# Another offset within 512 bytes for each split weight block of the second MoE

## The reference

```python
x = attention(q, k, v)          # 8 heads of 64, causal window of 128, ALiBi
x = soft_moe(x, phi, w1, w2)    # 32 slots: small products, all weights read once
# second MoE: every expert runs on every row
P = sinkhorn(exp(x @ w_gate - max), 8 rounds)
for e in range(8):
    h = np.maximum(x @ w1[e], 0.0)      # 512 -> 1024
    out += P[:, e:e + 1] * (h @ w2[e])  # 1024 -> 512
```

## Time and profile before

| what | value |
|---|---|
| median of 3 runs | 1057.57 us (1056.58 to 1058.82) |
| the profiled execution | 1057.44 us, its span 1055.5 us |
| mean granted TensorE clock | 0.969 of 2.4 GHz |
| TensorE matmul busy | 95% of the span |
| second MoE | from about 245 us to the end |

### The profile page before, as it was taken

The page is one execution under the profiler, slowest core; times in us unless marked ns, Lnnn a source line. Parts: engine busy times, 40 slices in busy tenths (PEclk is TensorE's granted clock), DMA queues, the critical chain, the costliest instruction groups (busy, mean ns, idle before and its releaser), DMA issues.

```text
span 1055.5 us, 25401 instructions
## 1 busy us (share of the span) xinstructions
PE 1005.1 (95%) x8599; PEld 924.3 (88%) x8599; DVE 748.2 (71%) x1994; ACT 583.7 (55%) x1368; POOL 615.1 (58%) x522
## 2 busy tenths in 40 slices
PE   7999979579999999999999999999999999999998
PEld 5888843029999999999999999999999999999998
DVE  7767741426898867876867778778768777877675
ACT  6777710224466746555655566466546564656552
POOL 6445410004487648684966596568747873877443
PEclk9999988658999999999999999999999999999999
DMA  5773267950200220022002200210040012000111
GB/s 184 262 277 112 71 273 265 408 209 2 81 1 2 81 81 2 2 82 81 2 3 83 81 2 2 99 63 1 14 148 5 2 72 91 2 2 20 61 41 61
DMA packets 36904, 87.81 MB, mean 83 GB/s; under 512 B 2976, under 2 KB 2976, under 8 KB 36768
## 3 DMA queue, kind: packets, MB, share of 16 engines
q1 hardware_dynamic: 36768, 86.07, 22.4%
HBM read 81.35 MB, written 4.72 MB: 82 GB/s over the span
## 4 chain that ended last, share of the span: by engine, by line
PE 41%; POOL 27%; issue 22%; DMA 4%; DVE 4%; ACT 1%; POOLq 1%; ACTq 0%; DVEq 0%
POOL s_split L499 19%; PE bank L775 8%; PE bank L777 7%; PE bank L779 7%; POOL t_split L504 4%; PE bank L568 3%; PE bank L578 3%; PE bank L597 3%; DMA late_raw<-slot_w_in 3%; PE bank L725 2%; PE bank L678 2%; PE bank L615 1%; POOL raw L533 1%; POOL raw L535 1%; POOL raw L537 1%
## 5 line engine op out<-in xcount | busy, mean ns | idle before, releaser
L499 POOL TENSOR_TENSOR s_split<-s_sum,s_split 128x512 fp32r<-128x512 f32 x288 | 372.5, 1309 | 342.2 <-ACT s_split L887 337.0
L1241 DVE SCALAR_TENSOR_TENSOR acc<-bank,gate_now,acc 128x256 f32<-128x256 f32 x441 | 228.6, 519 | 146.8 <-PE bank L779 145.8
L887 ACT ACTIVATE s_split<-s_sum 128x512 fp32r<-128x512 f32 x288 | 181.8, 632 | 247.6 <-PE bank L779 137.8
L775 PE MATMUL bank<-t_split,s_split 128*128 128x256 f32 x1008 | 284.2, 282 | 1.3 <-DVE acc L1235 1.1
L777 PE MATMUL bank<-t_split,s_split 128*128 128x256 f32 x1008 | 282.6, 280 | 0.0
L779 PE MATMUL bank<-t_split,s_split 128*128 128x256 f32 x1008 | 282.6, 280 | 0.0
L775 PEld LDWEIGHTS bank<-t_split,s_split 128*128 128x128 f32 x1008 | 189.4, 188 | 5.1 <-issue 3.4
L779 PEld LDWEIGHTS bank<-t_split,s_split 128*128 128x128 f32 x1008 | 192.6, 191 | 0.0
L777 PEld LDWEIGHTS bank<-t_split,s_split 128*128 128x128 f32 x1008 | 189.4, 188 | 0.0
L775 PE MATMUL bank<-t_split,a 128*128 128x256 f32 x576 | 164.1, 285 | 5.8 <-DVE acc L1235 2.5
L777 PE MATMUL bank<-t_split,a 128*128 128x256 f32 x576 | 162.6, 282 | 0.0
(11 more groups left out here) (167 smaller groups left out, 1952.5 us busy)
## 6 DMA issues: line engine op xcount, KB each, us to landing
raw<-big_w_in SPq DMA_DIRECT2D x15, 2048.0 KB, 8.6
early_raw<-slot_w_in SPq DMA_DIRECT2D x12, 1024.0 KB, 10.5
late_raw<-slot_w_in SPq DMA_DIRECT2D x10, 1024.0 KB, 13.5
slot_raw<-slot_w_in SPq DMA_DIRECT2D x7, 1024.0 KB, 5.2
q_ring<-q_tiles SPq DMA_DIRECT2D x18, 256.0 KB, 4.6
k_ring<-k_tiles SPq DMA_DIRECT2D x18, 256.0 KB, 4.9
v_ring<-v_rows SPq DMA_DIRECT2D x18, 256.0 KB, 2.7
out_rows<-acc SPq DMA_DIRECT2D x18, 256.0 KB, 2.0
```

Source lines behind the costliest of these rows:

```text
L499: pool.tensor_tensor(s_split[:, i, 1, :, :], s_sum[:, i, :, :], s_split[:, i, 0, :, :].bitcast(F32), ALU.subtract)\
L775: pe.matmul(to, left[:, 0, f, :], t_place(parity, k, 0)[:, f, :], start=(f == 0 and k in FRESH), stop=False, skip_group_check=k not in FRESH)
L887: act.activation(s_split[:, i, 0, :, :], s_sum[:, i, :, :], ACT.Copy).then_inc(s_hi_ready, 1)
L1241: done = dve.scalar_tensor_tensor(out=to, in0=got, scalar=gate, in1=to, op0=ALU.mult, op1=ALU.add)
```

## The change

Every block becomes a tensor of its own. In `t_split` each lies 16 floats (64 bytes) further than a gapless layout would have it, from `RAW_AT` itself on, so that the seven begin at 0, 64, 128, 192, 256, 320 and 384 bytes of the period. The three of `t_other` begin at 32, 288 and 480. No instruction, wait or shape changes: the same views are read and written at other addresses.

```diff
-        t_other, = place(OTHER_AT, RAW_AT, ("t_other", [P, len(DOUBLE), 2, HF, HD2], F32R))
-        t_split, = place(RAW_AT + PHASE, END + PHASE, ("t_split", [P, PRODUCTS, 2, HF, HD2], F32R))
+        BLOCK = 2 * HF * HD2
+        t_other = [place(OTHER_AT - PHASE + i * BLOCK + off, RAW_AT, (f"t_other{i}", [P, 2, HF, HD2], F32R))[0]
+                   for i, off in enumerate((8, 72, 120))]
+        t_split = [place(RAW_AT + i * (BLOCK + 16), END + PHASE, (f"t_split{i}", [P, 2, HF, HD2], F32R))[0] for i in range(PRODUCTS)]
...
             if i in DOUBLE and parity:
-                return t_other[:, DOUBLE.index(i), lo, :, :]
-            return t_split[:, i, lo, :, :]
+                return t_other[DOUBLE.index(i)][:, lo, :, :]
+            return t_split[i][:, lo, :, :]
```

## The result

| | kernel before | changed kernel |
|---|---|---|
| median | 1057.90 us (6 runs, 1056.02 to 1058.82) | 1063.67 us (6 runs, 1061.32 to 1067.61) |
| profiled execution | 1057.44 us, span 1055.5 | 1061.32 us, span 1059.3 |

The ratio is 1.0059, 95% interval 1.0039 to 1.0080: the changed kernel is slower, by 5.8 us at the median. Its runs spread over 6.3 us where those of before spread over 2.8, and the profiled execution is the lowest of them, so its trace shows 3.9 us of the 5.8.

What follows compares the result with a forecast made beforehand. TensorE's matmuls, one behind the other, were taken to bound the second MoE. Lost close stretches (2.4 us) plus wider spacing (4.5) made 6.9 us on 1057.44, giving 1064.3 us, range 1055 to 1082.

Steps and rivals of the forecast that it cites:

- both terms: The two nonzero parts of the sum: 2.4 us for lost close stretches and 4.5 us for wider spacing.
- step (c): Wide-pattern matmuls on the blocks: 6048 at 0.75 ns more each, as `hidden` at 320 shows, 4.5 us lost.
- Its own signs: Changed trace: only few 113.3 ns spacings running together, 422 to 424 matmuls per 50 us, TensorE waits under some 6 us.
- the 5.44 of the prediction: Behind `g_products`, the 48 matmuls were to take 5.65 us, not 5.44.
- What bounds the kernel: Second MoE: it takes as long as TensorE's matmuls one behind the other, so the distance of their starts counts.
- (a): ScalarE and GpSimd writing the blocks: no cost taken, being hidden by a whole pair of tiles; bounds none to 1.7 us.
- (b): Close stretches, mostly in expert 0 and behind `g_products`: none survives, 550 spacings lose 4.4 ns each, 2.4 us.
- the third rival: Some offset holds the close pattern: 4.4 ns gained per matmul, 1051.9 us with three blocks, 1033.2 with all; chance 0.16.
- A group at another offset tips them: Operand and weight streams reading SBUF: a group at another offset tips them from the closer to the wider pattern.
- Offset does nothing: The two patterns are a matter of timing alone and come as before, 1057.4 us; chance 0.20.
- Heavy offsets: Some offsets make the streams meet repeatedly: full step on half the blocks 1073.1 us, on all 1086.4; chance 0.24.

Runs made afterwards that it cites:

- the kernel at 0: All ten w2 blocks at offset 0, where the kernel before has them at 448; measured 1072.06 us, ratio 1.0140.

## Why the prediction was right

The forecast was 1064.3 us, measured 1063.67. What bounds the kernel and the direction of both terms held. That the number came so near is in part luck: step (c) took its price from a row that means something else, and the sum had no term for `hidden` itself (1.0 us less) nor for the gaps (0.8 less). The profiled execution, which the sum was made for, moved by 3.9 us of the forecast 6.9.

Its own signs were met only in part. There are runs of six to twelve spacings at 113.3, in T2; the windows have 424 and 426 starts, where 422 to 424 were expected; T2 of even experts stands 2.5 ns below the mean of all, by which step (c) was to be called wrong. Behind `g_products` the 48 matmuls took 5.74 us in expert 3 against 5.56 before: the 5.44 of the prediction leaves out their first, wide spacings. TensorE's waits, 5.2 us in all, stayed under 6, and no block lies above 120.0.

**What bounds the kernel.** Right: TensorE's pace alone moved, with other engines unchanged.

**(a) Writers, nothing.** Right: 1.045 and 2.412 us against 1.047 and 2.403, and TensorE's wait on them 1.2 us against 1.4.

**(b) The close stretches end, 2.4 us lost.** Right in substance, wrong in "no close stretch survives". In experts 1 to 7 the close spacings of before were worth about 1.5 us (354 of 5263 at 4.3 ns), and the changed kernel got 0.6 us of its own, in T2 of even experts, and 0.1 in T2 of odd ones behind `g_products`. That is the third rival come true in one place; one block in half of the experts was too little to decide. In expert 0 the spacings of 115 ns or less fell from 234 to 115, some 0.5 us.

**(c) Wider spacing, 4.5 us.** The size was near and the reason was not. Against a wide pattern of 117.76 the blocks at 0, 32, 256 and 288 cost 2.7 us in experts 1 to 7, those at 128 and 384 1.0, 64, 320 and 480 together 0.6: 4.3 us, where 0.75 x 5263 would be 3.9. But I took the price from `hidden` at 320 as that of "another offset", and 320 as such has none: B22 there pays one spacing of 122 and settles at 117.7, and blocks all of that class ran in 1052.9 us. The 118.5 of `hidden` was the price of changing over. The costly places were 0 and 32, for which the trace of before had no row. A mean of 0.75 ns over ten offsets, some better and some worse, met it by luck.

**What tips the pattern.** "A group at another offset tips them" was right: at the blocks' own offset `hidden` ended no close stretch. What I had not seen is the other direction, that a block at 128 sets the close pattern, and that `g_products` turns the pattern at 448 over, whichever it is.

**The rivals.** "Offset does nothing" fell with the kernel at 0, where nothing else differs from 448. So did the page that I set against the change: the Trainium skill, in "TensorE: Matmul & The Clock Gate", Part 2, has the next weights come through a port of their own without taking from the running matmul. The runs show 113.3 to 120.0 ns by nothing but the two operands' distance, so the next weights do not go by without a trace; whether it is at a port that they meet the moving operand, no run shows. "Heavy offsets" exist, at 120.0, but with 2.3 ns over 117.7, half of the step that I priced; on all blocks they gave 1072.1 and not 1086.

## What to carry to other kernels

Where every matmul has a weight load of its own beside the matmul ahead of it (here 128 columns of weights, recorded with 191 ns, against 256 moving ones every 113 to 120; no other form was tried), read the distance of the starts, not the durations, and look whether it has more than one value. If it has, try the byte distance between stationary and moving operands as a parameter of its own, for all matmuls of the stream at once: four matmuls at another distance, twice in 92, can hold all others in the slow pattern. Measure a survey of offsets with one offset per kernel; several in one kernel disturb each other at each change. Where an offset allows two patterns, one trace shows one mix of them: take several runs, and look at the granted clock of each before you compare single executions.

## What the runs showed of the hardware

- The spacing of matmuls of one shape (128 x 128 by 256 columns, float32r, full clock, a weight load each) is 113.3, 117.7 or 120.0 ns, or goes up and down between 115 and 122 with a mean of 117.3 to 118.7, by the distance of the operands modulo 256 bytes. Moving either operand does it (the stationary one in one kernel).
- At 64 and 192 there are two steady states, and a stream stays in one for hundreds of matmuls, until a gap, or a stream at another distance, disturbs it. At 192 the gap of `g_products` turned the state over each time in the kernel before (6 times) and with `c_stack` at 448 (6 times); at 64 it did so 3 times of 6.
- T1's twelve matmuls at distance 128 leave the stream in the close state at 192; the four of `hidden` turn it over.
- In some executions the granted clock fell to its half level for 15 or 16 matmuls in the middle of the second MoE, behind a gap of 1.8 to 2.5 us, which cost some 1.5 us; the same gaps in other executions were without it.
- Why this is so, whether two reads of SBUF meet or something else has this period, no run here tells apart. Distances that are not multiples of 32 bytes were not tried.
